# Attention over V in one full-precision matmul, or in three reduced-precision products with V and the probabilities split

## The chip, the cores and the metric

The kernel runs on one core of a Trainium2 chip. The metric is the device time of one execution in microseconds (us). The core has five engines that run their own instruction streams and meet only at semaphores: PE (matmuls, with its weight loads, PEld), DVE (vector), ACT (scalar), POOL (GpSimd) and SP, which here only issues DMAs.

## The reference

The program is an attention over chunks followed by two feed-forward networks. Cut to what matters here:

```python
for c in range(nc):                                   # chunks of 32 queries
    k_full = concat(mem_k, k[l_start:r_end])          # 8 memory rows + up to 56 rows
    v_full = concat(mem_v, v[l_start:r_end])
    scores = scale * q_c @ k_full.T
    a = exp(scores - max(scores)); a = a / (sum(a) + 1e-9)
    out[c] = a @ v_full                               # <- the product that is changed
x = out as (3072 tokens, 512)
g = s * relu(x @ w_in)**2 + b;   x2 = g @ w_out       # first network, d_ff 2048
g2 = h * sigmoid(1.702 h), h = x2 @ w_in2; out = g2 @ w_out2   # second network
```

There are 4 batches x 8 heads of 768 tokens with 64 channels each.

## The kernel before

Attention works on 32 query tiles of 96 tokens (`QT`). For each tile the 120 key rows of its window and the 8 memory rows make a context of 128. Two heads share one unit of work, since 2 x 64 channels fill 128 partitions: 4 units (`HP`) per tile, 128 units in all. Units 0 to 15 are done in a start-up of their own; the other 112 (from `FIRST` = 16) run hidden inside the first network, and only they are touched by the change.

The matmuls of the networks take three products in the type fp32r in place of one in fp32: each operand is split into a high part, which is the fp32 value converted to fp32r, and a low part, the value less the high part, and the products are high x high, high x low, low x high. ACT makes the high parts (`Copy` into an fp32r tile), DVE or POOL the low ones (a subtraction). In the steady attention, before the change, the scores are made in this way (`score`, L830, 3 matmuls of 256 columns), while the product with V is one fp32 matmul (`attend`, L853) of 192 columns (two heads x 96 tokens). In the trace an fp32 matmul is two records. The transposes (L817, L818, L841) are fp32 too.

The first network runs over token tiles `mm` 0 to 4, of 384, 384, 384, 480 and 480 tokens (`SIZES`). Each tile has 16 steps `f`. A step has 24 places: 12 matmuls of `first_product` (L885) and 12 of `second_product` of two steps earlier (L910 and L912). The table `AT` hangs the attention work onto these places. A unit n has a group of kind 1 and, some places later, one of kind 2; I call the two together a beat. PE in kind 1: transposes of the probabilities of unit n+1 (`transpose_probs`, L841), transposes of Q and K of unit n+4 (`transpose_qk`, L817 and L818). PE in kind 2: `attend(n)` and `score(n+3)`. There is about one beat per 19 places in tile 0, one per 16 in tiles 1 and 2, one per 12 (so two in a step) in tile 3, and one per 13.5 in tile 4 up to its ninth step.

ACT, in kind 1: `exp(n+2)` (L1071, two heads), `split_qk_hi(n+4)` (L1065, three pieces); in kind 2: `copy_x_hi(n)` (L1092 or L1097), and for units below 32 also `normalize` (L1078). Between them stand the step's own `nonlinear` (L1117, at place 12), `split_g_hi` (L1125) and in tile 0 `split_w_out_hi` (L1134). DVE in kind 1: `invert(n+2)` (L1412, L1416), `split_qk_lo(n+4)` (L1396, three pieces), `copy_pT(n+1)` (L1423, the transposed probabilities from PSUM to SBUF); in kind 2: `mask_and_max(n+3)` (L1405, two heads), `split_x_lo(n)` (L1428 or L1433); and the step's `gate` (L1458) and `split_g_lo` (L1464). POOL splits the weights in tile 0 (L646, L648, L653) and normalizes from unit 32 on (L695). Bank 6 of PSUM holds the transposed Q and K and the transposed probabilities, bank 7 the scores and the attention's output.

Every engine works its stream in order. `transpose_probs(n+1)` waits for the probabilities of its unit, for `pT_ready` of unit n (the copy out of bank 6) and for `qk_ready` of unit n+3 (the last L1396). SP issues the loads: Q and K of a tile (L471 to L474), V (`load_v`, L479 and L480) into one of two buffers `v_steady`, and the weights of tile 0 (L507, L516). `load_steady_v(j)` waits until the last unit of tile j-2 is attended, and what stands behind it in SP's queue waits with it.

## Time and profile before

| | us |
|---|---|
| median of 3 runs | 1174.82 (1174.70 to 1174.91) |
| the profiled execution | 1174.82 |
| its span, first to last instruction | 1173.0 |
| PE busy | 1162.9 (99%) |
| PE weight loads | 1016.2 (87%) |
| DVE busy | 905.1 (77%) |
| ACT busy | 670.8 (57%) |
| POOL busy | 348.6 (30%) |
| granted TensorE clock | 1.000 |

The profile is of one execution, whose own time is the median of the runs. Busy time of an engine is the union of its instructions; on PE an instruction's record lasts longer than the time until the next one may start, because the array is pipelined. So starts are compared below, not durations, where the pace of PE is meant. Steady attention lies between about 30 and 476 us; after it the two networks run alone.

### The profile page before, as it was taken

How to read it: one execution, taken by the hardware profiler on the slowest of the kernel's cores; microseconds unless marked ns; L12 is line 12 of the kernel's file. 1: busy time of each engine (PE TensorE's matmuls, PEld its weight loads, DVE VectorE, ACT ScalarE, POOL GpSimd, SP SyncE). 2: the span in 40 equal slices, each digit the busy share in tenths (PEclk: the TensorE clock that was granted, in tenths of full speed). 3: DMA queues.
4: the chain of work that ended last, by engine and by line, in shares of the span. 5: the costliest groups of instructions: out<-in, count | busy, mean ns of one | idle time of the engine just before them, and what ended most of it. 6: DMA issues, size and time to landing. Idle time of an engine off the chain costs nothing.

```text
span 1173.0 us, 19116 instructions
## 1 busy us (share of the span) xinstructions
PE 1162.9 (99%) x6058; PEld 1016.2 (87%) x6058; DVE 905.1 (77%) x2261; ACT 670.8 (57%) x1795; POOL 348.6 (30%) x356
## 2 busy tenths in 40 slices
PE   8999999999999999999999999999999999999998
PEld 5899999999988888888888888888888888888887
DVE  6788877878887887668898877879577878677663
ACT  6788766767766766345446554447344556444452
POOL 3754111111111111324642134640246421244300
PEclk9999999999999999999999999999999999999999
DMA  7753322322242231113424434124233234222231
GB/s 151 166 134 77 78 57 58 78 57 51 52 81 66 50 99 36 37 36 107 144 75 123 123 106 141 57 76 140 77 104 126 76 106 133 82 71 73 73 116 63
DMA packets 167689, 104.26 MB, mean 89 GB/s; under 512 B 99495, under 2 KB 144039, under 8 KB 167591
## 3 DMA queue, kind: packets, MB, share of 16 engines
q1 hardware_dynamic: 166368, 102.82, 32.5%
q8 instruction: 50, 0.82, 0.3%
q14 instruction: 48, 0.39, 0.1%
q10 hardware_dynamic: 1223, 0.23, 0.1%
HBM read 89.26 MB, written 13.76 MB: 88 GB/s over the span
## 4 chain that ended last, share of the span: by engine, by line
PE 95%; ACT 2%; DVE 1%; DMA 1%; issue 0%; POOL 0%; SPq 0%; POOLq 0%; DVEq 0%
PE psum L953 26%; PE psum L910 22%; PE psum L912 22%; PE psum L885 14%; PE psum L830 3%; PE psum L853 3%; PE psum L841 2%; PE psum L818 1%; DMA result<-in_moe_w_out_dram 1%; PE psum L817 1%; PE psum L752 1%; ACT arena_raw L1071 0%; PE psum L789 0%; PE psum L779 0%; ACT arena_raw L1078 0%
## 5 line engine op out<-in xcount | busy, mean ns | idle before, releaser
L953 PE MATMUL psum<-weights 128*128 128x512 f32 (+1 forms) x1344 | 337.6, 386 | 0.0
L953 PEld LDWEIGHTS psum<-weights 128*128 128x128 f32 x1344 | 252.3, 188 | 49.1
L912 PE MATMUL psum<-g_hi,weights 128*128 128x384 f32 (+1 forms) x768 | 223.3, 363 | 0.0
L885 PE MATMUL psum<-arena,weights 128*128 128x384 f32 (+1 forms) x960 | 215.7, 360 | 0.0
L1501 DVE TENSOR_TENSOR arena_raw<-psum,arena_raw 128x512 f32<-128x512 f32 (+1 forms) x160 | 109.0, 681 | 85.6 <-PE psum L953 83.7
L885 PEld LDWEIGHTS psum<-arena,weights 128*128 128x128 f32 x960 | 166.3, 188 | 8.8 <-DVE ffn L1458 0.2
L695 POOL TENSOR_TENSOR arena_raw<-arena_raw,small 96x256 f32<-96x256 f32 x96 | 58.6, 610 | 302.8 <-DVE small L1416 302.8
L912 PEld LDWEIGHTS psum<-g_hi,weights 128*128 128x128 f32 x768 | 139.3, 188 | 8.8
L912 PE MATMUL psum<-g_lo,weights 128*128 128x384 f32 (+1 forms) x384 | 138.2, 360 | 0.0
L910 PE MATMUL psum<-weights,g_hi 128*128 128x512 f32 x384 | 118.2, 389 | 0.0
L665 POOL TENSOR_TENSOR arena_raw<-arena_raw 128x256 f32<-128x256 f32 x32 | 27.2, 851 | 305.7 <-DMA arena_raw<-in_moe_w_in_dram 187.7
L1187 ACT ACTIVATE arena_raw<-arena_raw 128x512 f32<-128x512 f32 x48 | 30.4, 633 | 128.6 <-DVE arena_raw L1501 128.6
L1396 DVE TENSOR_TENSOR arena<-psum,arena 128x96 fp32r<-128x96 f32 x336 | 82.9, 274 | 24.8 <-ACT arena L1065 20.6
L1071 ACT ACTIVATE arena_raw<-arena_raw,small 96x128 f32<-96x128 f32 x224 | 87.4, 392 | 25.2 <-DVE small L1405 25.1
L658 POOL TENSOR_TENSOR weights<-arena_raw,weights 128x512 fp32r<-128x512 f32 x48 | 69.1, 1453 | 86.1 <-ACT weights L1146 86.1
L910 PEld LDWEIGHTS psum<-weights,g_hi 128*128 128x128 f32 x384 | 72.1, 188 | 15.0
L1471 DVE TENSOR_TENSOR weights<-arena_raw,weights 128x1024 fp32r<-128x1024 f32 x64 | 83.5, 1305 | 0.0
L1146 ACT ACTIVATE weights<-arena_raw 128x512 fp32r<-128x512 f32 x96 | 58.5, 625 | 39.4 <-PE psum L910 26.7
L1065 ACT ACTIVATE arena<-psum 128x96 fp32r<-128x96 f32 x336 | 75.0, 257 | 4.1 <-PE psum L818 1.6
L912 PEld LDWEIGHTS psum<-g_lo,weights 128*128 128x128 f32 x384 | 72.1, 188 | 5.5
L910 PE MATMUL psum<-weights,g_lo 128*128 128x512 f32 x192 | 74.7, 389 | 0.0
L910 PE MATMUL psum<-weights,arena 128*128 128x512 f32 x288 | 74.5, 389 | 0.0
(129 smaller groups left out, 2124.3 us busy)
## 6 DMA issues: line engine op xcount, KB each, us to landing
arena_raw<-in_moe_w_out_dram SPq DMA_DIRECT2D x128, 256.0 KB, 4.0
arena_raw<-in_moe_w_in_dram SPq DMA_DIRECT2D x64, 256.0 KB, 3.1
arena_raw<-in_k_dram SPq DMA_DIRECT2D x31, 240.0 KB
arena_raw<-in_v_dram SPq DMA_DIRECT2D x30, 240.0 KB
arena_raw<-x_scratch SPq DMA_DIRECT2D x3, 2048.0 KB, 10.5
arena_raw<-in_q_dram SPq DMA_DIRECT2D x31, 192.0 KB
out_dram<-result SPq DMA_DIRECT2D x5, 1024.0 KB, 5.1
result<-in_moe_w_in_dram SPq DMA_DIRECT2D x16, 256.0 KB, 4.2
```

The source lines that it names most:

```text
L658: nc.gpsimd.tensor_tensor(lo, w_out_raw(k), hi.bitcast(F32), ALU.subtract).then_inc(w_out2_now_ready, 1)
L695: nc.gpsimd.tensor_tensor(probs[:, n % 2, :, :], probs[:, n % 2, :, :], inv_total[:, n % 2, :].unsqueeze(2).to_broadcast([QT, 2, P]), ALU.mult
L885: last = nc.tensor.matmul(dst, w[:, kt * P:(kt + 1) * P], x, start=(kt + i == 0), stop=(kt == KT - 1 and i == 2))
L910: last = nc.tensor.matmul(acc[c][:, :], g[:, piece], w, start=start, stop=stop)
L912: last = nc.tensor.matmul(acc[c][:, 0:n], w[:, piece], g, start=start, stop=stop)
L953: last = nc.tensor.matmul(bank_of[bank][:, 0:width(i)], w[:, k * P:(k + 1) * P], x[:, k, :], start=(k + t == 0), stop=(k == 1 and t == 2))
L1065: last = nc.scalar.activation(qk_hi[parts, n % 2, cols], bank_qk[parts, source], ACT.Copy)
L1071: nc.scalar.activation(probs[:, n % 2, h, :], probs[:, n % 2, h, :], ACT.Exp, scale=-1.0, bias=exp_bias[:, n % 2, h:h + 1], accum_out=tota ...
L1146: nc.scalar.activation(hi, w_out_raw(k), ACT.Copy).then_inc(w_out2_hi_done, 1)
L1396: last = nc.vector.tensor_tensor(qk_lo[parts, n % 2, cols], bank_qk[parts, source], qk_hi[parts, n % 2, cols].bitcast(F32), ALU.subtract)
L1471: last = nc.vector.tensor_tensor(rows_parts(q, 1)[:, these], rows_raw[:, these], rows_parts(q, 0)[:, these].bitcast(F32), ALU.subtract)
L1501: return nc.vector.tensor_tensor(to[:, 0:w], bank_of[bank][:, 0:w], other[:, 0:w], ALU.add)
```

## The change

The product with V is done as the scores are: V and the transposed probabilities are split into high and low parts, and `attend` issues three fp32r matmuls of 192 columns in place of one fp32 matmul.

- V is loaded into one raw buffer, `v_raw`. POOL splits it: `split_v(j)` is a conversion of 128x512 and a subtraction of 128x512 per query tile, 28 tiles in all. It stands in POOL's stream once ahead of the tiles, and then once per tile at kind 1 of the unit with n % 4 == 1, behind `normalize(n+2)` where there is one.
- ACT gets one more instruction per unit, `split_pT_hi(n+1)`, 128x192 from PSUM, behind `split_qk_hi(n+4)` in kind 1.
- DVE's `copy_pT` becomes `split_pT_lo`, a subtraction of the same size. `split_qk_lo(n+4)` now waits for `pT_hi_done` of unit n+1 as well.
- `max_ready` is raised once per unit, not once per head, and `exp` waits for it ahead of both heads.
- SP: `load_steady_v(j)` waits for `v_ready` of tile j-1 (the split of the tile before, by POOL) in place of `attended` of tile j-2; the very first one waits for `s_attended` 6.

Cut to its core, the diff is:

```diff
-        pT = raw_area(ATTN + 4480, 384).rearrange("p (a c) -> p a c", a=2)
-        v_steady = raw_area(ATTN + 5248, 1024).rearrange("p (a c) -> p a c", a=2)
+        pT_hi = area(ATTN + 4480, 384).rearrange("p (a c) -> p a c", a=2)
+        pT_lo = area(ATTN + 4864, 384).rearrange("p (a c) -> p a c", a=2)
+        v_hi = area(ATTN + 5248, 1024).rearrange("p (a c) -> p a c", a=2)
+        v_lo = area(ATTN + 6272, 1024).rearrange("p (a c) -> p a c", a=2)
...
             def load_steady_v(j):
-                if HP * (j - 2) >= FIRST:
-                    sp.wait_ge(attended, nth(HP * (j - 1) - 1))
-                load_v(j, v_steady[:, j % 2, :], v_loaded[j % 2])
+                if HP * (j - 1) < FIRST:
+                    sp.wait_ge(s_attended, 2 * ((FIRST // HP - 1) // 2 * 2 + 1))
+                else:
+                    sp.wait_ge(v_ready, nth(HP * j - 1) // HP)
+                load_v(j, v_raw, v_loaded)
...
+            def split_v(j):
+                i = j - FIRST // HP
+                pool.wait_ge(v_loaded, 32 * (i + 1))
+                if i >= 2:
+                    pool.wait_ge(attended, nth(HP * (j - 1) - 1))
+                nc.gpsimd.tensor_copy(v_hi[:, j % 2, :], v_raw).then_inc(v_hi_done, 1)
+                pool.wait_ge(v_hi_done, i + 1)
+                nc.gpsimd.tensor_tensor(v_lo[:, j % 2, :], v_raw, v_hi[:, j % 2, :].bitcast(F32), ALU.subtract
+                                        ).then_inc(v_ready, 1)
...
+            split_v(FIRST // HP)
...
                         for kind, n in AT.get(pos, ()):
+                            j = n // HP + 1
                             if kind == 1 and there(n + 2) and pool_normalizes(n + 2):
                                 normalize(n + 2)
+                            if kind == 1 and n % HP == 1 and there(HP * j) and j > FIRST // HP:
+                                split_v(j)
...
                 if hp == 0:
-                    pe.wait_ge(v_loaded[j % 2], 32 * ((j - FIRST // HP) // 2 + 1))
+                    pe.wait_ge(v_ready, j - FIRST // HP + 1)
                 pe.wait_ge(pT_ready, nth(n))
-                nc.tensor.matmul(bank_o, v_steady[:, j % 2, hp * P:(hp + 1) * P], pT[:, n % 2, :], start=True, stop=True
-                                 ).then_inc(attended, 1)
+                for i, (a, c) in enumerate(((v_hi, pT_hi), (v_hi, pT_lo), (v_lo, pT_hi))):
+                    last = nc.tensor.matmul(bank_o, a[:, j % 2, hp * P:(hp + 1) * P], c[:, n % 2, :],
+                                            start=(i == 0), stop=(i == 2))
+                last.then_inc(attended, 1)
...
+            def split_pT_hi(n):
+                if there(n + LEAD - 1):
+                    act.wait_ge(qk_transposed, nth(n + LEAD - 1))
+                act.wait_ge(probs_transposed, nth(n))
+                nc.scalar.activation(pT_hi[:, n % 2, :], bank_pT, ACT.Copy).then_inc(pT_hi_done, 1)
             def exp(n):
+                act.wait_ge(max_ready, nth(n))
                 for h in range(2):
-                    act.wait_ge(max_ready, 2 * nth(n) - 1 + h)
...
             def split_qk_lo(n):
                 dve.wait_ge(qk_hi_done, nth(n))
+                if there(n - LEAD + 1):
+                    dve.wait_ge(pT_hi_done, nth(n - LEAD + 1))
...
-            def copy_pT(n):
-                if there(n + LEAD - 1):
-                    dve.wait_ge(qk_transposed, nth(n + LEAD - 1))
-                dve.wait_ge(probs_transposed, nth(n))
-                nc.vector.tensor_copy(pT[:, n % 2, :], bank_pT).then_inc(pT_ready, 1)
+            def split_pT_lo(n):
+                dve.wait_ge(pT_hi_done, nth(n))
+                nc.vector.tensor_tensor(pT_lo[:, n % 2, :], bank_pT, pT_hi[:, n % 2, :].bitcast(F32), ALU.subtract
+                                        ).then_inc(pT_ready, 1)
```

ACT's stream in a step of tile 3, from the step's `nonlinear` over its second beat. Before:

```order
L1117 ACTIVATE ffn<-psum 128x480 [waits hid_ready]
L1071 ACTIVATE arena_raw,small<-arena_raw,small 96x128 [waits max_ready] x2
L1065 ACTIVATE arena<-psum 128x96 [waits qk_transposed]
L1065 ACTIVATE arena<-psum 64x128 x2
L1092 ACTIVATE result<-psum 64x96 [waits result_stored,attended,scored]
```

and after, where L1149 is L1117 of before, L1101 is L1071, L1088 is L1065, L1122 is L1092, and L1096 is `split_pT_hi`:

```order
L1149 ACTIVATE ffn<-psum 128x480 [waits hid_ready]
L1101 ACTIVATE arena_raw,small<-arena_raw,small 96x128 [waits max_ready]
L1101 ACTIVATE arena_raw,small<-arena_raw,small 96x128
L1088 ACTIVATE arena<-psum 128x96 [waits qk_transposed]
L1088 ACTIVATE arena<-psum 64x128 x2
L1096 ACTIVATE arena<-psum 128x192 [waits probs_transposed,qk_transposed]
L1122 ACTIVATE result<-psum 64x96 [waits result_stored,attended,scored]
```

One instruction came in between L1065 and the copy of the attention's output.

DVE's stream in a beat of a tile of 384 tokens. Before:

```order
L1412 TENSOR_SCALAR small<-small 96x2 [waits exp_done]
L1416 RECIPROCAL small<-small 96x2 [waits probs_ready,total_ready]
L1396 TENSOR_TENSOR arena<-psum,arena 128x96 [waits qk_hi_done]
L1396 TENSOR_TENSOR arena<-psum,arena 64x128 x2
L1423 COPY arena_raw<-psum 128x192 [waits probs_transposed,qk_transposed]
L1464 SCALAR_TENSOR_TENSOR g_lo<-ffn,columns,g_hi 128x384 [waits g_hi_done]
```

and after:

```order
L1446 TENSOR_SCALAR small<-small 96x2 [waits exp_done]
L1450 RECIPROCAL small<-small 96x2 [waits probs_ready,total_ready]
L1430 TENSOR_TENSOR arena<-psum,arena 128x96 [waits pT_hi_done,qk_hi_done]
L1430 TENSOR_TENSOR arena<-psum,arena 64x128 x2
L1454 TENSOR_TENSOR arena<-psum,arena 128x192 [waits pT_hi_done]
L1496 SCALAR_TENSOR_TENSOR g_lo<-ffn,columns,g_hi 128x384 [waits g_hi_done]
```

The number and the places of the instructions are the same; the first subtraction, and with it all behind it, now stands behind ACT's new instruction.

POOL's stream where tile 0 begins. Before:

```order
L646 CAST weights<-result 128x512 [waits w_in_loaded0]
L648 TENSOR_TENSOR weights<-result,weights 128x512 [waits w_hi_first_in]
L646 CAST weights<-result 128x512 [waits w_in_loaded1]
L648 TENSOR_TENSOR weights<-result,weights 128x512 [waits w_hi_first_in]
L653 TENSOR_TENSOR weights<-result,weights 128x512 [waits w_hi_out]
```

and after:

```order
L653 CAST weights<-result 128x512 [waits w_in_loaded0]
L655 TENSOR_TENSOR weights<-result,weights 128x512 [waits w_hi_first_in]
L705 CAST arena<-arena_raw 128x512 [waits v_loaded]
L707 TENSOR_TENSOR arena<-arena_raw,arena 128x512 [waits v_hi_done]
L653 CAST weights<-result 128x512 [waits w_in_loaded1]
L655 TENSOR_TENSOR weights<-result,weights 128x512 [waits w_hi_first_in]
L660 TENSOR_TENSOR weights<-result,weights 128x512 [waits w_hi_out]
```

The two instructions of the first V stand between the second and the third piece of `w_in` that POOL converts.

## Rows read from the trace of the kernel before

**Rows 1.** The page: the chain that ended last, share of the span by engine.

```profile
PE 95%; ACT 2%; DVE 1%; DMA 1%; issue 0%; POOL 0%; SPq 0%; POOLq 0%; DVEq 0%
```

**Rows 2.** By stage (tile 0; tiles 1 and 2; tile 3); (x) counts.

```profile
core 0: us, PE busy (x) PEld busy (x) DVE busy (x) ACT busy (x) POOL busy (x), PEclk, DMA share, GB/s
30.00:113.00 83.00, 80.13 (x510) 76.04 (x511) 66.67 (x237) 67.72 (x234) 49.31 (x46) 1.00 0.57 133
113.00:305.00 192.00, 192.00 (x1246) 190.11 (x1246) 155.11 (x657) 131.68 (x509) 30.16 (x50) 1.00 0.29 60
305.00:427.00 122.00, 121.53 (x705) 108.03 (x704) 100.29 (x423) 82.00 (x321) 20.46 (x34) 1.00 0.34 72
```

**Rows 3.** Timeline, tile 2: start us, us, engine, line, tiles, count.

```profile
251.45 0.49 PE L853 MATMUL psum<-arena_raw 128*128 128x192 f32 x2
...
251.64 0.65 PE L830 MATMUL psum<-arena 128*96 128x256 f32 x3
251.84 0.36 DVE L1423 COPY arena_raw<-psum 128x192 f32<-128x192 f32 x1
...
252.13 0.69 PE L885 MATMUL psum<-arena,weights 128*128 128x384 f32 x3
```

**Rows 4.** Timeline, tile 0: scores without a product with V before them.

```profile
41.83 0.52 PE L830 MATMUL psum<-arena 128*96 128x256 f32 x3
...
42.19 0.34 PE L912 MATMUL psum<-g_lo,weights 128*128 128x384 f32 x1
```

**Rows 5.** Timeline, start-up: weight loads of fp32r matmuls of 128 columns.

```profile
15.76 0.58 PEld L779 LDWEIGHTS psum<-arena 64*96 64x96 f32 x12
```

**Rows 6.** Single lines, weight loads: duration ns min/median/max, first and last start, forms.

```profile
L779 PEld LDWEIGHTS psum<-arena x96: 156/162/162, 7.3 to 27.5; 64*96 64x96 f32 x96
...
L912 PEld LDWEIGHTS psum<-g_hi,weights x768: 187/188/193, 40.8 to 674.0; 128*128 128x128 f32 x192
```

**Rows 7.** Timeline, tile 3: the second beat of a step.

```profile
343.89 0.57 ACT L1117 ACTIVATE ffn<-psum 128x480 f32<-128x480 f32 x1 [1.06 <-PE psum L885]
...
345.12 0.68 ACT L1065 ACTIVATE arena<-psum 128x96 fp32r<-128x96 f32 x3
...
346.62 0.36 DVE L1423 COPY arena_raw<-psum 128x192 f32<-128x192 f32 x1
...
347.11 0.38 PE L912 MATMUL psum<-g_lo,weights 128*128 128x480 f32 x1
347.20 0.14 PEld L841 LDWEIGHTS psum<-ident,arena_raw 96*128 96x128 f32 x1
...
347.23 0.28 DVE L1405 CUSTOM_DVE_ANT_0 arena_raw<-psum,masks 96x128 f32<-96x128 f32 x1
```

**Rows 8.** Single lines of the start-up that have the size of the new ones.

```profile
L1059 ACT ACTIVATE arena<-psum x8: 306/310/332, 15.4 to 34.0; 128x192 fp32r<-128x192 f32 x8
...
L1390 DVE TENSOR_TENSOR arena<-psum,arena x8: 356/358/360, 15.8 to 34.4; 128x192 fp32r<-128x192 f32 x8
```

**Rows 9.** Timeline, tile 2: the transposes behind the copy of rows 3.

```profile
253.36 0.33 PEld L841 LDWEIGHTS psum<-ident,arena_raw 96*128 96x128 f32 x2
```

**Rows 10.** Timeline, tile 0: ACT, and PE behind it.

```profile
98.67 0.50 ACT L1097 ACTIVATE arena<-psum 64x96 fp32r<-64x96 f32 x2
...
99.95 0.20 PEld L841 LDWEIGHTS psum<-ident,arena_raw 96*128 96x128 f32 x2 [0.38 <-ACT arena_raw L1078]
```

**Rows 11.** What SP waited for up to 120 us: us, times, longest.

```profile
SPq L479 <- PE psum L853: 37.8, 4, 13.7
```

**Rows 12.** Timeline, end of tile 0: the first unit that POOL normalizes.

```profile
112.19 0.61 POOL L695 TENSOR_TENSOR arena_raw<-arena_raw,small 96x256 f32<-96x256 f32 x1 [0.29 <-DVE small L1416]
...
114.03 0.32 PEld L841 LDWEIGHTS psum<-ident,arena_raw 96*128 96x128 f32 x2
```

**Rows 13.** Timeline, tile 0: a small DVE instruction beside one of POOL.

```profile
41.20 1.28 POOL L653 TENSOR_TENSOR weights<-result,weights 128x512 fp32r<-128x512 f32 x1
41.23 1.28 DVE L1412 TENSOR_SCALAR small<-small 96x2 f32<-96x2 f32 x1 [0.42 <-ACT arena_raw L1071]
```

More of the change, by code:

```diff
@@ L324, in bass_chunked_attention_two_ffn @@
         s_v_loaded = [sem("s_v_loaded0"), sem("s_v_loaded1")]
-        v_loaded = [sem("v_loaded0"), sem("v_loaded1")]
+        v_loaded = sem("v_loaded")
+        v_hi_done = sem("v_hi_done")
+        v_ready = sem("v_ready")
         w_in_loaded = [sem("w_in_loaded0"), sem("w_in_loaded1")]
@@ L357, in bass_chunked_attention_two_ffn @@
         probs_transposed = sem("probs_transposed")
+        pT_hi_done = sem("pT_hi_done")
         pT_ready = sem("pT_ready")
@@ L825, in score @@
                 if there(n - 1):
-                    pe.wait_ge(max_ready, 2 * nth(n - 1))
+                    pe.wait_ge(max_ready, nth(n - 1))
                 if there(n - LEAD):
@@ L848, in attend @@
                 if there(n + LEAD - 2):
-                    pe.wait_ge(max_ready, 2 * nth(n + LEAD - 2))
+                    pe.wait_ge(max_ready, nth(n + LEAD - 2))
                 if hp == 0:
-                    pe.wait_ge(v_loaded[j % 2], 32 * ((j - FIRST // HP) // 2 + 1))
+                    pe.wait_ge(v_ready, j - FIRST // HP + 1)
                 pe.wait_ge(pT_ready, nth(n))
-                nc.tensor.matmul(bank_o, v_steady[:, j % 2, hp * P:(hp + 1) * P], pT[:, n % 2, :], start=True, stop=True
-                                 ).then_inc(attended, 1)
+                for i, (a, c) in enumerate(((v_hi, pT_hi), (v_hi, pT_lo), (v_lo, pT_hi))):
+                    last = nc.tensor.matmul(bank_o, a[:, j % 2, hp * P:(hp + 1) * P], c[:, n % 2, :],
+                                            start=(i == 0), stop=(i == 2))
+                last.then_inc(attended, 1)
             def group(kind, n):
@@ L1107, in group @@
                         split_qk_hi(n + LEAD)
+                    if there(n + 1):
+                        split_pT_hi(n + 1)
                 else:
@@ L1404, in mask_and_max @@
                 for h in range(2):
-                    nc.vector.tensor_tensor_reduce(
+                    last = nc.vector.tensor_tensor_reduce(
                         out=probs[:, n % 2, h, :], in0=bank_s[0:QT, h * P:(h + 1) * P], in1=masks[:, mask_of(n // HP), :],
-                        scale=-SCALE, scalar=-MASKED, op0=ALU.add, op1=ALU.min, accum_out=exp_bias[:, n % 2, h:h + 1]
-                        ).then_inc(max_ready, 1)
+                        scale=-SCALE, scalar=-MASKED, op0=ALU.add, op1=ALU.min, accum_out=exp_bias[:, n % 2, h:h + 1])
+                last.then_inc(max_ready, 1)
             def invert(n):
@@ L1445, in group @@
                     if there(n + 1):
-                        copy_pT(n + 1)
+                        split_pT_lo(n + 1)
                 else:
```

## The prediction

> **What bounds the kernel now.** I read the chain that ended last first. It is PE for 95% of the span [rows 1], so a microsecond that PE gains or loses is one of the result. Then the busy time by stage [rows 2]. While attention runs beside tiles 1 and 2, PE is busy for 192.00 of 192 us, in tile 3 for 121.53 of 122, and in tile 0 for 80.13 of 83. ACT is busy there for 131.68, 82.00 and 67.72 us, and DVE for 155.11, 100.29 and 66.67, which is about 80%. The granted clock is 1.00 in all of them, its higher level. So PE is the bound and the others feed it, with little room left. What the change is worth is therefore two things: what the three products take on PE, and whether ACT's new instruction makes a wait of PE's longer. After 480 us nothing of it is left in the program.
>
> **PE: the products.** One product with V and one group of scores take from 251.45 to 252.13, 0.68 us [rows 3]. Scores alone take from 41.83 to 42.19, 0.36 us, or 120 ns for each fp32r matmul of 256 columns [rows 4]. So the fp32 product costs 0.32 us. The new one is three fp32r matmuls of 192 columns with 128 columns of weights, a form that the trace does not have. By their columns they would start every 90 ns (192/256 of 120). But each has a weight load of its own. The start-up's matmuls stream 128 columns over a load of 96 columns, in pairs on the two halves of the rows: 12 loads in 0.58 us, the last lasting 0.162. That is 0.418 us over five pair intervals, 84 ns each [rows 5, 6], where their columns would give 60. There the load sets the pace. A load of 128 columns lasts 188 ns against 162 [rows 6], 26 ns more, so I expect 110 ns between starts. Behind the third comes a load of only 96 columns, so 90 ns. Together 110 + 110 + 90 = 310 ns against 320: 10 ns saved, x 112 units = 1.1 us. The bounds are 3 x 90 = 270 ns (5.6 us saved) and, since a matmul of 256 columns takes no more than 120, 3 x 120 = 360 (4.5 us lost). I take 310, nearest to the row of the small matmuls.
>
> A load of 128 columns of fp32r lasts 26 ns longer than one of 96 [rows 6], in line with its width and with no sign of a faster way at the full width. The Trainium skill, page "TensorE: Matmul & The Clock Gate", section "Weight-path perf modes — Fast Weight Load (FWL) and DoubleRow", has weights of exactly 128 columns load about twice as fast where the type is not FP32. By that rule the load would hide and the product would cost 270 ns, 5.6 us saved in all; the trace's row speaks against it for fp32r.
>
> **ACT and DVE.** `split_pT_hi` has the size of the start-up's L1059: 0.31 us. `split_pT_lo` has that of L1390, 0.358 us [rows 8], against 0.36 for the copy that it replaces [rows 3]. So DVE's own work stays, but all of its L1396 and what follows moves back by 0.31 us, since the first L1396 now waits for ACT's new instruction. What waits behind it on DVE is the last part of the beat: L1396, the low part, and then the maxima of the next unit. PE waits for these at L841.
>
> In tile 3 there is no room for it. ACT starts the second beat when PE's products release L1117 at 343.89. L1065 runs from 345.12 to 345.80 behind it, DVE's copy ends at 346.98, and the load of L841 starts at 347.20. The copy's end is thus passed on in 0.22 us. PE's last matmul ahead began at 347.11 and one of 480 columns takes about 0.22 more, so PE came to L841 at 347.33 [rows 7]: the room is 0.13 us at most, and I take 0.1. This repeats in each of the 16 steps of the tile. The wait starts from PE's own products of the same step, so nothing makes up for it in the next: 16 x (0.31 - 0.10) = 3.4 us. Bounds: 0, if ACT makes up for it, and 16 x 0.31 = 5.0.
>
> In tiles 1 and 2 the copy ends at 252.20 [rows 3] and L841's load starts at 253.36 [rows 9]: 1.16 us, less 0.22 for passing it on, leaves 0.94. The change wants 0.31, and 0.21 for `exp`, which now waits for the second head's maximum too (one head's pass is recorded at 0.28 [rows 7], and the two overlap a little). This is hidden. For the two beats behind the result copies, where DVE is late, and for tile 4, I add 0.4 us; bounds 0 and 2.
>
> In tile 0 ACT also normalizes and splits `w_out`, and PE waits for the normalizing: L1097 from 98.67, and its load for L841 waits 0.38 us for that, until 99.95 [rows 10]. ACT is busy for 67.72 of 83 us [rows 2] and gets 17 x 0.31 = 5.3 more. I take 8 of the 17 beats as having no idle time of ACT in them: 2.5 us, and 0.4 for two in which `exp` starts late. Bounds 0 and 5.3 + 0.8.
>
> **POOL and SP.** `split_v` has a subtraction of the size of L653, 1.28 us [rows 13], and a conversion that I take at half of it, as it reads one input: 1.9 us per query tile. From tile 1 on POOL is idle for 162 of 192 us [rows 2], and V is wanted three beats later: nothing. At one place it counts. The split of the ninth query tile stands between the last L653, which ends 0.29 us ahead of 112.19, and the first L695 [rows 12]. L695 then ends near 111.90 + 1.9 + 0.61 = 114.4, while PE loads for L841 at 114.03: 0.5 us late, once. On SP, `load_v` waited for PE for 37.8 us in all, up to 13.7 at a time, with the loads of weights behind it [rows 11]. The new wait, for a split that stands about 1.5 beats ahead in the program, is shorter where POOL is early. I take 0.4 us as gained in tile 0 (0 to 1.5), since the PE waits there are partly for late `w_out`.
>
> **The sum.** -1.1 (products) + 3.4 (tile 3) + 0.4 + 2.5 + 0.4 + 0.5 - 0.4 = +5.7 us. The profiled execution took 1174.82 us (span 1173.0), which is also the median, so 1180.5 us. This case's own range is 1177.5 to 1185.
>
> **Rivals.**
> 1. The three products run at their columns' pace, 270 ns, and the waits come as above. -5.6 in place of -1.1: 1176.0 us. For it: PE loads ahead of time everywhere else. Against it: the 84 ns of rows 5.
> 2. Faster: the products at 270 ns, and the waits do not appear, because ACT has 30 to 40% of idle time and starts its beat earlier than I think. Then 1174.8 - 5.6 + 0.7 (what is left in tile 0) = 1169.9 us. Decided where L841 waits in tile 3: below 0.05 us per step. Against it: L1065 there is back to back with the work ahead of it.
> 3. DVE is held by POOL. A DVE instruction of two elements lasts 1.28 us beside a POOL subtraction, almost start to end [rows 13]. `split_v` adds 28 such subtractions, most of them where POOL was idle. If 10 of them catch a small DVE instruction or L1464 and push it by 0.9 us of which 0.7 reaches PE, 7 us more: 1187.5 us. For it: rows 13. Against it: in tiles 1 and 2 there is 0.4 us of room left, and `split_v` follows L695, when DVE works from PSUM.
> 4. Tile 0 is starved of weights: the splits of V and SP's new first waits delay `w_in` by 2 us more than I think, and PE waits 3 us or more: 1184 us.
>
> The wait on L1412 of rows 13 is what the Trainium skill describes on its page "SBUF — State Buffer", section "SBUF: two separate sides", as the port pair that DVE and GpSimd take in turns, each for a whole instruction. The trace agrees (1.28 us beside 1.28), and the rule gives nothing for the sum beyond rival 3.
>
> **Chances.** My forecast 0.50, rival 1 0.17, rival 2 0.14, rival 3 0.12, rival 4 0.07. A measurement can tell 0.2% from no change, 2.35 us here. Slower than 1177.2: 0.45 of mine, all of rivals 3 and 4, and 0.03 of rival 1: 0.67. Within: 0.05 + 0.14 = 0.19. Faster: 0.14. For the range I reach to rival 3 above and to just short of rival 2 below: 1171 to 1189 us.
>
> **What would show it.** The new matmuls' weight loads should start 110 ns apart; 90 speaks for rivals 1 and 2, 120 or more against my step on PE. In tile 3 the L841 of the second beat should start 0.2 us later against the matmul ahead of it, and the stretch from the tile's first to last matmul should be 3.4 us longer. In tiles 1 and 2 PE should keep a busy share of 100% and their stretch shrink by 0.5 us (48 x 10 ns). In tile 0 the idle time of PE should grow by about 3 us. Stretched instructions L1412 and L1464 in tiles 1 to 3, now at their plain durations, would show rival 3. I am wrong if tile 3 does not get longer, or if the products' pace is off by more than 15 ns.

## The result, and the profile after

The changed kernel takes 1192.37 us (median of 4 runs, 1191.92 to 1192.62) against 1174.87 for the kernel before on the same chip: 1.47% slower, ratio 1.0147 with the interval 1.013 to 1.0165. Its profiled execution took 1191.04 us, span 1189.2. My 1180.5 had the direction and missed two thirds of the size; the time lies outside my range.

The page of the changed kernel: busy time, and the chain that ended last, which answers to [rows 1].

```profile
PE 1170.7 (98%) x6170; PEld 1010.4 (85%) x6170; DVE 895.9 (75%) x2261; ACT 698.6 (59%) x1907; POOL 401.2 (34%) x412
...
PE 85%; ACT 6%; DVE 4%; issue 3%; POOL 1%; DVEq 0%; ACTq 0%; POOLq 0%
```

PE's share of the chain falls from 95% to 85%. ACT and DVE have taken seven of these ten points and `issue` three, though ACT's busy share only went from 57 to 59% and DVE's fell from 77 to 75%. It is their order that the kernel waits for, not their load. By stage, with windows moved to where the stages now lie; this answers to [rows 2].

```profile
core 0: us, PE busy (x) PEld busy (x) DVE busy (x) ACT busy (x) POOL busy (x), PEclk, DMA share, GB/s
30.00:114.00 84.00, 80.20 (x524) 75.74 (x525) 65.27 (x236) 70.36 (x248) 57.19 (x55) 1.00 0.57 132
114.00:312.00 198.00, 195.76 (x1293) 186.28 (x1292) 150.84 (x654) 142.19 (x550) 53.43 (x75) 1.00 0.27 60
312.00:440.00 128.00, 123.18 (x729) 104.96 (x728) 94.61 (x422) 90.63 (x354) 34.72 (x49) 1.00 0.28 66
```

The clock is at its higher level as before. PE, which had no gap in tiles 1 and 2, has 2.2 us of them now, and 4.8 in tile 3 (0.5 before). A better measure is how late `transpose_probs` (L841, now L862) of a given unit starts. Unit 33, at the end of tile 0, starts at 120.09 us against 118.77; unit 81, at the end of tile 2, at 311.39 against 303.62; unit 113, at the end of tile 3, at 435.49 against 420.27. So tile 0 costs 1.3 us, tiles 1 and 2 cost 6.5 in their 48 beats, tile 3 costs 7.4 in its 32, and the rest 0.9. I had 3.0, 0.4 (with tile 4) and 3.4. This one execution is 1.3 us faster than the median; no trace shows where the others lose that.

The groups of ACT and DVE in tiles 1 and 2, first before (118 to 305 us), then after (ACT from 118 to 312, DVE from 118 to 305): busy time, mean of one | idle time ahead of them and what ended it.

```profile
L1405 DVE CUSTOM_DVE_ANT_0 arena_raw<-psum,masks 96x128 f32<-96x128 f32 x98 | 24.4, 284 | 11.9 <-ACT arena L1097 9.0 <-ACT result L1092 1.6
L1071 ACT ACTIVATE arena_raw<-arena_raw,small 96x128 f32<-96x128 f32 x98 | 38.2, 391 | 8.1 <-DVE small L1405 8.1
L1097 ACT ACTIVATE arena<-psum 64x96 fp32r<-64x96 f32 x72 | 17.6, 244 | 30.6 <-PE psum L830 30.1
```

```profile
L1439 DVE CUSTOM_DVE_ANT_0 arena_raw<-psum,masks 96x128 f32<-96x128 f32 x94 | 23.0, 280 | 0.1
L1101 ACT ACTIVATE arena_raw<-arena_raw,small 96x128 f32<-96x128 f32 x96 | 37.8, 395 | 44.4 <-DVE small L1439 44.4
L1127 ACT ACTIVATE arena<-psum 64x96 fp32r<-64x96 f32 x74 | 18.0, 243 | 2.5 <-PE psum L851 1.8
L1430 DVE TENSOR_TENSOR arena<-psum,arena 128x96 fp32r<-128x96 f32 x141 | 35.0, 275 | 32.3 <-ACT arena L1096 31.5
```

These lines tell most of the case. Before, `copy_x_hi` on ACT waited 30.6 us for PE's scores, and the maxima 11.9 us, most of them for that copy, so in the end for PE as well. Now DVE hardly waits ahead of the maxima (0.1 us), and ACT and DVE wait for each other: `exp` 44.4 us for the maxima, `split_qk_lo` 32.3 us for `split_pT_hi`. A beat of tile 2:

```profile
243.72 0.28 DVE L1439 CUSTOM_DVE_ANT_0 arena_raw<-psum,masks 96x128 f32<-96x128 f32 x1
...
244.26 0.40 ACT L1101 ACTIVATE arena_raw<-arena_raw,small 96x128 f32<-96x128 f32 x1 [0.81 <-DVE small L1439]
...
245.05 0.67 ACT L1088 ACTIVATE arena<-psum 128x96 fp32r<-128x96 f32 x3
245.17 0.47 PE L875 MATMUL psum<-arena 128*128 128x192 f32 x3
...
245.48 0.52 PE L851 MATMUL psum<-arena 128*96 128x256 f32 x3
...
245.74 0.33 ACT L1096 ACTIVATE arena<-psum 128x192 fp32r<-128x192 f32 x1
245.84 1.56 PE L908 MATMUL psum<-arena,weights 128*128 128x384 f32 x8
...
246.17 0.76 DVE L1430 TENSOR_TENSOR arena<-psum,arena 128x96 fp32r<-128x96 f32 x3 [0.59 <-ACT arena L1096]
...
246.96 0.36 DVE L1454 TENSOR_TENSOR arena<-psum,arena 128x192 fp32r<-128x192 f32 x1
247.23 0.28 DVE L1439 CUSTOM_DVE_ANT_0 arena_raw<-psum,masks 96x128 f32<-96x128 f32 x1
247.39 0.20 PEld L862 LDWEIGHTS psum<-ident,arena_raw 96*128 96x128 f32 x2 [0.31 <-issue]
```

It is a ring: maxima (243.72), `exp` (244.26), high Q and K (245.05), high probabilities (245.74), low Q and K (246.17), low probabilities (246.96), and at once the maxima of the next unit (247.23). PE's transposes hang on it. In two of three beats a `split_g_lo` or a `gate` stands between the low probabilities and the next maxima besides; this is the third. In numbers, the change lengthens the ring by 0.22 us for `exp` (it starts 0.54 us behind the maxima; 0.32 in `b1_act` of the next section, where it waits for one head) and by 0.42 at `split_pT_hi` (from the end of the last L1088, 245.72, to L1430 at 246.17; before, from L1065's end, 239.49, to 239.51). The lines of `b1_act`, and those of the kernel before:

```profile
241.36 0.28 DVE L1417 CUSTOM_DVE_ANT_0 arena_raw<-psum,masks 96x128 f32<-96x128 f32 x1
...
241.68 0.40 ACT L1079 ACTIVATE arena_raw<-arena_raw,small 96x128 f32<-96x128 f32 x1 [0.68 <-DVE small L1417]
```

```profile
238.81 0.68 ACT L1065 ACTIVATE arena<-psum 128x96 fp32r<-128x96 f32 x3
...
239.51 0.76 DVE L1396 TENSOR_TENSOR arena<-psum,arena 128x96 fp32r<-128x96 f32 x3
```

### The profile page after: what moved, and what is told of

It is laid out like the page before. It is cut to its first block, busy times and chain, and to the rows that moved or that the text cites. A ratio compares the mean times of both kernels' runs of the same rounds, so it can differ in the third digit from the quotient of the medians.

```text
span 1189.2 us, 19643 instructions
## 1 busy us (share of the span) xinstructions
PE 1170.7 (98%) x6170; PEld 1010.4 (85%) x6170; DVE 895.9 (75%) x2261; ACT 698.6 (59%) x1907; POOL 401.2 (34%) x412
## 4 chain that ended last, share of the span: by engine, by line
PE 85%; ACT 6%; DVE 4%; issue 3%; POOL 1%; DVEq 0%; ACTq 0%; POOLq 0%
PE psum L976 25%; PE psum L933 22%; PE psum L935 18%; PE psum L908 11%; PE psum L851 2%; PE psum L875 2%; DVE arena L1430 2%; ACT arena_raw L1101 2%; PE psum L862 2%; ACT arena L1088 2%; ACT arena L1096 1%; PE psum L839 1%; DVE arena L1454 1%; PE psum L838 1%; PE psum L773 1%
## 5 line engine op out<-in xcount | busy, mean ns | idle before, releaser
L908 PE MATMUL psum<-arena,weights 128*128 128x384 f32 (+1 forms) x960 | 215.9, 360 | 0.2 <-DVE ffn L1490 0.2
L908 PEld LDWEIGHTS psum<-arena,weights 128*128 128x128 f32 x960 | 166.4, 188 | 9.1 <-DVE ffn L1490 0.4
L712 POOL TENSOR_TENSOR arena_raw<-arena_raw,small 96x256 f32<-96x256 f32 x96 | 58.6, 610 | 271.7 <-DVE small L1450 261.3
L1430 DVE TENSOR_TENSOR arena<-psum,arena 128x96 fp32r<-128x96 f32 x336 | 83.2, 275 | 68.3 <-ACT arena L1096 65.9
L1101 ACT ACTIVATE arena_raw<-arena_raw,small 96x128 f32<-96x128 f32 x224 | 88.0, 394 | 78.0 <-DVE small L1439 77.6
L1088 ACT ACTIVATE arena<-psum 128x96 fp32r<-128x96 f32 x336 | 74.7, 256 | 2.3
```

The source lines that it names most:

```text
L712: nc.gpsimd.tensor_tensor(probs[:, n % 2, :, :], probs[:, n % 2, :, :], inv_total[:, n % 2, :].unsqueeze(2).to_broadcast([QT, 2, P]), ALU.mult
L908: last = nc.tensor.matmul(dst, w[:, kt * P:(kt + 1) * P], x, start=(kt + i == 0), stop=(kt == KT - 1 and i == 2))
L1088: last = nc.scalar.activation(qk_hi[parts, n % 2, cols], bank_qk[parts, source], ACT.Copy)
L1101: nc.scalar.activation(probs[:, n % 2, h, :], probs[:, n % 2, h, :], ACT.Exp, scale=-1.0, bias=exp_bias[:, n % 2, h:h + 1], accum_out=tota ...
L1430: last = nc.vector.tensor_tensor(qk_lo[parts, n % 2, cols], bank_qk[parts, source], qk_hi[parts, n % 2, cols].bitcast(F32), ALU.subtract)
```

## The experiments

Four theories. **Ring**: what is added to the ring is paid once its room, the time that a turn has to spare against PE's beat, is used up. **Exp wait**: the wait for both heads is the price. **POOL**: `split_v` slows DVE down. **Products**: they are slower than thought. The table at the end of this section has where each kernel lost its time. Each time is compared with the kernel before on the same chip. The diffs are cut to the lines that matter, some of their conditions left out, and comments in them are mine.

**Parts put on the kernel before.** `b1_act`: ACT's operation and DVE's wait alone.

```diff
+            def copy_pT_spare(n):   # behind split_qk_hi(n + LEAD) in kind 1
+                act.wait_ge(probs_transposed, nth(n))
+                nc.scalar.activation(pT_spare[:, n % 2, :], bank_pT, ACT.Copy).then_inc(pT_hi_done, 1)
             def split_qk_lo(n):
+                    dve.wait_ge(pT_hi_done, nth(n - LEAD + 1))
             def copy_pT(n):
+                dve.wait_ge(pT_hi_done, nth(n))
```

> The kernel before, with one thing added: ACT's Copy of the transposed probabilities (128x192 from PSUM, into a place that nobody reads) behind split_qk_hi in kind 1, and DVE's split_qk_lo and copy_pT wait for it. V, the product and the two max_ready waits are as before. Ring theory (the extra ACT operation and its hand-over lengthen the closed loop maxima, exp, high Q and K, low Q and K, copy, next maxima by about 0.4 us a beat, and what a beat is late the next beat inherits): most of the 17.5 us returns here, +10 to +15 us on the kernel before, about 1185 to 1190. If exp's wait for both heads is the main price: +3 us or less. If POOL's work beside DVE is the price: 0. If the room of 0.94 us per beat hid it, as my prediction had it: +3 to +6, nearly all of it in tiles 0 and 3.

1183.59 us, +9.0 (ratio 1.0078, 1.0063 to 1.0093): just short of the ring's +10, above the others'. Nearly all of it is in tiles 0 (2.1) and 3 (5.9), with only 0.7 in tiles 1 and 2. That is where my prediction's room of 0.94 us would have put it too, so this run alone does not decide.

`b2_once`: the wait of `exp` alone.

```diff
-                    act.wait_ge(max_ready, 2 * nth(n) - 1 + h)
+            act.wait_ge(max_ready, nth(n))   # once, and max_ready raised once per unit
```

> The kernel before, with one thing changed: max_ready is raised once per unit behind the second head, and exp waits for it ahead of both heads. Ring theory: exp starts up to one maximum (0.31 us) later only where it had waited for the first head; in the kernel before the loop in tiles 1 and 2 still had room of about 0.5 us a beat, so +1 to +3 us, mostly in tile 3. If the exp wait is the main price of the change: +8 or more. If the waits are nothing and POOL or PE's pace is the price: 0.

1176.32, +1.7 (1.0005 to 1.0024). This is not the main price by itself. Its trace has all of it in tile 0, not in tile 3 as I expected.

`b3_pool`: POOL's conversion and subtraction per tile alone (`split_v` of the change, into `v_spare`).

```diff
+                nc.gpsimd.tensor_copy(v_spare[:, 0, :], v_steady[:, j % 2, :]).then_inc(v_hi_done, 1)
+                nc.gpsimd.tensor_tensor(v_spare[:, 1, :], v_steady[:, j % 2, :], v_spare[:, 0, :].bitcast(F32), ALU.subtract).then_inc(v_ready, 1)
```

> The kernel before, with POOL's two operations of 128x512 per query tile added (conversion and subtraction into places that nobody reads), at the places where the change puts split_v, and SP waits for them ahead of the load that would overwrite their input. Nothing else waits for them. Ring theory: 0 to +2 us, since only POOL's own queue is later (its normalize, once per tile, by up to 1 us). Rival, POOL's reads and writes slow DVE down: +7 us or more, and DVE's busy time up.

1177.09, +2.5 (1.001 to 1.003), a little above the ring's window and far from the rival's. Nearly all of it is in tile 0; in tiles 1 to 3 nothing. Yet its trace shows the contention there:

```profile
250.94 1.29 POOL L704 TENSOR_TENSOR arena<-arena_raw,arena 128x512 fp32r<-128x512 f32 x1
251.14 1.50 DVE L1482 SCALAR_TENSOR_TENSOR g_lo<-ffn,columns,g_hi 128x384 fp32r<-128x384 f32 x1
```

`split_g_lo` lasts 1.50 us in place of 0.62 and ends 0.41 us behind POOL's subtraction. The room swallows it: none of the four such places in tiles 1 and 2 makes a transpose late.

`b4_act_once`: both of the first two.

> The kernel before with both additions to the loop together: ACT's extra Copy with DVE waiting for it, and exp waiting for both heads. PE's product with V is still one fp32 matmul and POOL has no more work. Ring theory: the loop is as long as in the changed kernel and only the products' small gain is missing, so 1190 to 1195, the changed kernel's 1192.4 within 3 us. If the rest of the change (V split on POOL, three products, the later loads by SP) has a share of its own, it is short of that by this share: 1183 or less.

1199.09, +24.5 (1.0194 to 1.0224). The parts alone are +9.0 and +1.7; together they are more than twice their sum, and more than the whole change. That they don't add up speaks for a ring with room: in tiles 1 and 2 they cost 0.7 and 0.0 alone and 9.3 together. But I had expected no more than 1195, so something in the changed kernel must give 7 us back.

**Parts taken from the changed kernel.** `a1_heads`: `exp` waits head by head again.

> The changed kernel with max_ready raised per head again and exp waiting head by head. Ring theory: the loop is shorter by 0.1 to 0.2 us a beat where exp waits, so 1186 to 1189. If the exp wait is the main price of the change: 1180 or less. If POOL contention or the products are the price: 1192, no change.

1182.66, 9.7 us back, where I had thought of 3 to 6. Tiles 1 and 2 lose only 0.3 now, tile 3 still 5.8. The same wait that costs 1.7 us on the kernel before is worth 9.7 here.

`a3_pT_first`: ACT's order.

```diff
+                    if there(n + 1):
+                        split_pT_hi(n + 1)
                     if there(n + 2) and there(n):
                         exp(n + 2)
                     if there(n + LEAD) and there(n):
                         split_qk_hi(n + LEAD)
-                    if there(n + 1):
-                        split_pT_hi(n + 1)
```

> The changed kernel with ACT's split_pT_hi(n+1) moved ahead of exp(n+2) and split_qk_hi(n+4) in kind 1. ACT idles about 0.8 us there, waiting for the maxima, and the transposed probabilities are usually ready by then. Ring theory: the 0.33 us and its hand-over leave the loop, so most of the loss is back: 1174 to 1181. If the maxima wait no longer for it but exp's wait for both heads or POOL is the price: above 1187. If the probabilities are transposed too late for it, exp is held up by it and the kernel is slower than 1192.

1178.83 (1.0025 to 1.0055): 13.5 us back by moving one ACT instruction into ACT's idle time. The ring theory's window.

`a5_first_heads`: both.

> The changed kernel with both: split_pT_hi ahead of exp in ACT's stream, and exp waiting head by head. Ring theory: the loop is then as long as in the kernel before but for a DVE subtraction in place of a copy, and PE has the products' gain of 1.1 us less POOL's and the start's cost: 1173 to 1178. If something outside the loop costs, it stays above 1180.

1178.38, just outside. Tiles 1 and 2 are 0.4 us faster than before, tile 3 loses 2.8. There the transposes are as late as the maxima:

```profile
352.77 0.20 PEld L862 LDWEIGHTS psum<-ident,arena_raw 96*128 96x128 f32 x2 [0.25 <-issue]
...
353.09 0.28 DVE L1439 CUSTOM_DVE_ANT_0 arena_raw<-psum,masks 96x128 f32<-96x128 f32 x1
...
353.43 0.33 ACT L1096 ACTIVATE arena<-psum 128x192 fp32r<-128x192 f32 x1
...
353.64 0.40 ACT L1101 ACTIVATE arena_raw<-arena_raw,small 96x128 f32<-96x128 f32 x1
```

`exp` is held until 353.64 by `split_pT_hi`, 0.55 us behind the maxima and not 0.32.

`a8_first_both`: DVE's low part moved up as well.

```diff
+                if there(n - LEAD):   # split_qk_hi: bank 6 is read by one engine at a time
+                    act.wait_ge(pT_ready, nth(n - LEAD + 1))
+                    if there(n + 1):   # DVE, kind 1: ahead of invert and split_qk_lo
+                        split_pT_lo(n + 1)
```

> As the last one, and DVE's split_pT_lo(n+1) stands ahead of invert(n+2) and split_qk_lo(n+4) as well, so that both halves of the split fall under exp; ACT's split_qk_hi then waits for it, since both read bank 6. Ring theory: the split of the probabilities leaves the loop altogether, which is then shorter than in the kernel before by the copy's 0.33 us a beat: 1171 to 1175, below the kernel before's 1174.9. If bank 6's order becomes the bound (split_qk_hi late behind the low part), 1178 or more.

1180.04, a miss on the ring theory's side, and in the range of its rival, the order of bank 6: in tile 3 `split_qk_hi` now idles 7.5 us in all for `split_pT_lo`. No further run tested this.

**The 7 us that were unexplained.** In `b4_act_once` the operation ahead of the maxima is a copy, in the changed kernel a subtraction of the same duration. `c1_two_operands` is `b4_act_once` with one line changed (below), and `c3_one_operand` the changed kernel with a copy in place of the subtraction, so that it leaves the low part of the probabilities out.

```diff
-                nc.vector.tensor_copy(pT[:, n % 2, :], bank_pT).then_inc(pT_ready, 1)
+                nc.vector.tensor_tensor(pT[:, n % 2, :], bank_pT, pT_spare[:, n % 2, :].bitcast(F32), ALU.max).then_inc(pT_ready, 1)
```

> The kernel before with ACT's extra Copy, DVE's wait for it and exp's wait for both heads (the one that took 1199.1), and DVE's copy_pT now made by a tensor_tensor of two operands (the larger of the value and ACT's copy of it) in place of tensor_copy. In the traces DVE's next instruction starts 0.03 us after a tensor_copy's end but 0.09 us before a tensor_tensor's end, so the loop should be 0.12 us a beat shorter: where it is saturated (48 beats of tiles 1 and 2, 30 of tile 3) that is about 9 us, so 1188 to 1192. If the form of the operation is nothing and the 6.7 us between that kernel and the changed one lie in the three products or the V split, it stays at 1197 or more.

> The changed kernel with DVE's split_pT_lo made by a tensor_copy in place of the subtraction (the low part of the probabilities is left out). By the same 0.12 us a beat in 78 saturated beats: 1199 to 1203, slower by 7 to 10 us with one operand less. If the form is nothing: 1192.

1187.99 and 1202.22: 11.1 us less and 9.8 more, as expected. DVE in `b4_act_once` and in `c1_two_operands`:

```profile
250.51 0.36 DVE L1436 COPY arena_raw<-psum 128x192 f32<-128x192 f32 x1
250.89 0.29 DVE L1417 CUSTOM_DVE_ANT_0 arena_raw<-psum,masks 96x128 f32<-96x128 f32 x1
```

```profile
246.03 0.36 DVE L1436 TENSOR_TENSOR arena_raw<-psum,arena 128x192 f32<-128x192 f32 x1
246.30 0.28 DVE L1417 CUSTOM_DVE_ANT_0 arena_raw<-psum,masks 96x128 f32<-96x128 f32 x1
```

From start to start these are 0.38 against 0.27 us. `q1_v_copy` makes POOL's second operation a copy in the changed kernel, and so leaves the low part of V out:

```diff
-                nc.gpsimd.tensor_tensor(v_lo[:, j % 2, :], v_raw, v_hi[:, j % 2, :].bitcast(F32), ALU.subtract
+                nc.gpsimd.tensor_copy(v_lo[:, j % 2, :], v_raw).then_inc(v_ready, 1)
```

> The changed kernel with the second of POOL's operations per tile a tensor_copy in place of the subtraction (the low part of V is left out). In the changed kernel's trace split_g_lo of DVE, both of whose inputs are in SBUF, takes 1.18 to 1.33 us in place of 0.62 in the four places of tiles 1 and 2 where POOL's subtraction runs beside it, and PE is 0.8 us later behind each. If that is a cause: 3 us or so less, 1188 to 1190. If it is absorbed as it is where POOL's work was added to the kernel before: 1191 to 1193. If POOL's contention is the main price: 1185 or less.

1188.52, 3.9 us less. First the changed kernel, then this one:

```profile
254.52 1.29 POOL L707 TENSOR_TENSOR arena<-arena_raw,arena 128x512 fp32r<-128x512 f32 x1
...
254.90 1.33 DVE L1496 SCALAR_TENSOR_TENSOR g_lo<-ffn,columns,g_hi 128x384 fp32r<-128x384 f32 x1
256.15 0.28 DVE L1439 CUSTOM_DVE_ANT_0 arena_raw<-psum,masks 96x128 f32<-96x128 f32 x1
```

```profile
254.99 0.63 DVE L1495 SCALAR_TENSOR_TENSOR g_lo<-ffn,columns,g_hi 128x384 fp32r<-128x384 f32 x1
255.54 0.28 DVE L1438 CUSTOM_DVE_ANT_0 arena_raw<-psum,masks 96x128 f32<-96x128 f32 x1
```

So POOL's contention is a real cause here, where the ring has no room, and costs nothing in tiles 1 to 3 of `b3_pool`. In tiles 1 and 2 of the changed kernel four of the twelve subtractions of V hold up a `split_g_lo`. Behind each of these four the transposes get 0.76 to 0.88 us later, against 0.18 to 0.20 at the same places without the subtraction: 2.5 us of the 3.9. A fifth, at 474.36 us in tile 4, costs 0.7.

`p1_products`: the products alone on the kernel before, all three with the high parts (the low parts are left out), and one conversion per tile on POOL for V.

```diff
-                nc.tensor.matmul(bank_o, v_steady[:, j % 2, hp * P:(hp + 1) * P], pT[:, n % 2, :], start=True, stop=True
+                for i in range(3):
+                    last = nc.tensor.matmul(bank_o, v_hi[:, j % 2, hp * P:(hp + 1) * P], pT[:, n % 2, :], start=(i == 0), stop=(i == 2))
```

> The kernel before with the product with V made by three fp32r matmuls of 192 columns (three times high V by high probabilities, low parts left out); DVE's copy_pT writes fp32r, POOL makes V's high part by one conversion per tile, PE waits for that. ACT, exp's waits and DVE's order are those before. Both theories of the loop: the products' gain of 10 ns a unit, 1.1 us in all, and up to 1 us of POOL's work in tile 0 against it, so 1173.5 to 1175.5. If the three products carry a share of the loss: above 1177.

1173.48, -1.0 (ratio 0.9993, 0.9984 to 1.0003, so not clear of zero). The products are no part of the loss.

**Operands or partitions.** Still open was why a copy costs 0.12 us more. The four kernels here change only the order of the three pieces in DVE's `split_qk_lo`. The third piece starts at partition 64.

```diff
-                for (parts, cols), source in QK_PIECES:
+                for (parts, cols), source in QK_PIECES[2:] + QK_PIECES[:2]:
```

> The kernel before with ACT's extra Copy, DVE's wait for it and exp's wait for both heads, DVE's copy still with one operand (the 1199.1 us kernel), but DVE's split_qk_lo does its three pieces in the order third, first, second, so that the last one before the copy starts at partition 0 and not at 64. If the 0.12 us behind the copy come from its one operand, only the copy's own start is earlier: 1190 to 1194. If they come from the partition where the last SBUF operand began (the copy reads none, so the maxima are compared with the piece at partition 64), both go, 0.23 us a beat: no loss left in tiles 1 and 2 and 4 us in tile 3, 1181 to 1185.

> The changed kernel with only that order of split_qk_lo's pieces. split_pT_lo then starts 0.1 us earlier against the piece ahead of it. Loop theory: 0.1 us a beat off a loop that is 0.13 us too long in tiles 1 and 2 and 0.24 in tile 3, so 7 to 8 us less, 1183 to 1186. If the order of the pieces is nothing: 1192.

> The changed kernel with split_pT_hi ahead of exp, exp waiting head by head (the 1178.4 us kernel), and that order of the pieces. It lost 2.8 us in tile 3, 0.09 us a beat, and gained 0.4 in tiles 1 and 2. Loop theory: the 0.1 us a beat takes the loss in tile 3 away, 1175 to 1176.5, as fast as the kernel before within what can be measured. If tile 3 is held by ACT or by the order of bank 6 instead: 1177.5 or more.

> The kernel before with only that order of the pieces. Its loop has room in every tile, so a shorter one gives nothing: within 0.5 us of the kernel before. If its loop were the bound in tile 3: 1 to 3 us less.

`d4_act_once_order` took 1178.66 with the one-operand copy: 20.4 us less than `b4_act_once`, more even than I expected. DVE there:

```profile
240.56 0.76 DVE L1408 TENSOR_TENSOR arena<-psum,arena 64x128 fp32r<-64x128 f32 x3 [0.59 <-ACT arena L1074]
241.24 0.34 DVE L1436 COPY arena_raw<-psum 128x192 f32<-128x192 f32 x1
241.50 0.27 DVE L1417 CUSTOM_DVE_ANT_0 arena_raw<-psum,masks 96x128 f32<-96x128 f32 x1
```

Copy and maxima both start before their predecessor's record ends: 0.26 us from start to start. It was not the number of operands but the partition at which the last one from SBUF began; the second operand of `c1_two_operands` begins at partition 0, and that is how it helped. `d2_after_order`: 1182.29, 10.1 us less than the changed kernel and a little more than expected. `d1_first_order`: 1174.97, ratio 1.0004 (0.9995 to 1.0013): the whole loss gone, with the change's arithmetic complete. POOL's split, its meetings with `split_g_lo` and SP's new waits are all still in this kernel, so they cost nothing that can be measured once the ring has room. `d3_before_order`: 1173.23, ratio 0.999 (0.9981 to 0.9999), the fastest of these kernels (its product with V is the one of the kernel before). Against my expectation of 0.5 us at most it gained 1.4; 0.7 of that had come by the end of tile 0 and 0.4 in tile 3, too little to be sure of a cause.

Time lost against the kernel before (starts of the transposes of units 33, 81 and 113 and the end, in one profiled execution of each):

| us | tile 0 | tiles 1, 2 | tile 3 | rest |
|---|---|---|---|---|
| the changed kernel | 1.3 | 6.5 | 7.4 | 0.9 |
| b1_act | 2.1 | 0.7 | 5.9 | -0.1 |
| b2_once | 1.6 | 0.0 | 0.1 | 0.0 |
| b3_pool | 2.8 | 0.0 | -0.1 | 0.8 |
| b4_act_once | 2.7 | 9.3 | 11.5 | 0.7 |
| a1_heads | 0.9 | 0.3 | 5.8 | 0.6 |
| a3_pT_first | 1.4 | -0.3 | 2.8 | 0.1 |
| a5_first_heads | 1.0 | -0.4 | 2.8 | 0.1 |
| a8_first_both | 0.5 | 0.8 | 3.6 | 0.2 |
| c1_two_operands | 1.8 | 3.8 | 7.6 | 0.0 |
| c3_one_operand | 3.9 | 11.3 | 11.5 | 1.5 |
| q1_v_copy | 2.6 | 4.1 | 7.5 | 0.2 |
| p1_products | -1.2 | -0.4 | -0.1 | -0.2 |
| d4_act_once_order | -0.7 | 0.4 | 4.0 | 0.0 |
| d2_after_order | 0.5 | 1.9 | 4.2 | 0.8 |
| d1_first_order | -0.1 | -0.5 | 0.6 | 0.1 |
| d3_before_order | -0.7 | 0.0 | -0.4 | 0.0 |

One number for the room makes the column of tiles 1 and 2. Their 48 beats lose 0.194 us each in `b4_act_once`, where 0.42 + 0.22 = 0.64 is added: room 0.45. In `c1_two_operands` 0.64 - 0.11 = 0.53 is added and 0.079 lost: 0.45. In `b1_act` 0.42 is added and next to nothing lost. And `d4_act_once_order` adds 0.64 - 0.22 = 0.42 and loses 0.01. These are means: `b4_act_once` mostly loses about 0.3 us in two of three beats and less than 0.1 in the third.

## Why the prediction was wrong, step by step

- **Products, -1.1 us: right.** In the beat above L875 starts at 245.17 and L851 at 245.48, 0.31 us as worked out. Product and scores together take 0.67 us, up to L908 at 245.84, against 0.68 before [rows 3]. `p1_products` gained 1.0, within the noise.
- **Tiles 1 and 2, "this is hidden", +0.4: the step that failed.** The 0.52 us that I took as wanted is close to what the runs show (0.53), but that is luck: I had 0.31 for ACT and 0.21 for `exp`; it is 0.42 and 0.22, less 0.11 that the subtraction gives back. The room was not 0.94 us but 0.45. I read it where PE waits, from the end of the copy to the load of L841 [rows 3, 9]. But DVE starts the next maxima as soon as the copy is done, and from them the next copy follows through `exp` and the splits, so the room is that of the whole ring. The row that shows it was there: in tiles 1 and 2 of the kernel before DVE idled 11.9 us ahead of the maxima, 0.24 a beat, well below the 0.52 wanted. The other half of the room lies mostly ahead of `exp`. By the mean starts of all beats of tiles 1 and 2, the maxima came 1.03 us behind the copy before and 0.75 in `b4_act_once`, which is 0.27 of room; `exp` came 0.46 behind the maxima where 0.32 would have done, since ACT was often not free, which is 0.13 more; and 0.03 lay ahead of `split_qk_hi`: 0.44 in all. What is missing in one beat is passed to the next, and so 0.08 us became 3.8 in the 48 beats of `c1_two_operands`. The changed kernel loses 6.5 there, 2.5 of them by POOL's contention.
- **Tile 3, +3.4: mechanism right, size half.** From one beat [rows 7] I took 0.31 us added, a room of 0.1 and one late beat per step, 0.21 a step. "Nothing makes up for it in the next" holds, and so does the one late beat: but for the first step the changed kernel loses 0.33 to 0.47 us in one of a step's two beats and at most 0.13 in the other. The term that was mis-sized is what is added. `exp` waits for the second head here as well, which I had left out of this tile, and `split_pT_hi` costs 0.42 us and not 0.31: with the 0.11 back, 0.53 is added. My own sum would then give 16 x (0.53 - 0.10) = 6.9; lost are 7.4 us, 0.46 a step. A room of 0.1 is itself only rough: `b1_act` and `d4_act_once_order` both add 0.42 and lose 5.9 and 4.0, and I cannot say why they differ.
- **Rival 3, POOL's contention, 0.12: a true part.** I priced it at 7 us with 10 meetings; it is 3.9, of which the traces show 3.2: 2.5 from four meetings in tiles 1 and 2, and 0.7 from the one in tile 4. My argument against it, 0.4 us of room left, fell with the room. The Trainium skill, page "SBUF — State Buffer", section "Who interferes with whom", says that a DVE instruction with two SBUF inputs contends with one of POOL that reads SBUF, and that one with at most one does not, outside the modes that use two ports. The traces agree: L1496 has two and lasts 1.33 us. L1490, with one of its inputs in PSUM, keeps its 0.61 us at the four places of tiles 1 and 2 where POOL's subtraction runs beside all of it.
- **Tile 0, +3.0: too much**, 1.3 in the profiled execution (2.6 in that of `q1_v_copy`, which has the same ring). Rival 4, a tile 0 that loses 3 us or more beyond this, did not show. The one place that I named came as told, `split_v` between the last weight split and L712, with PE 0.40 us late:

```profile
113.58 1.30 POOL L707 TENSOR_TENSOR arena<-arena_raw,arena 128x512 fp32r<-128x512 f32 x1
114.84 0.61 POOL L712 TENSOR_TENSOR arena_raw<-arena_raw,small 96x256 f32<-96x256 f32 x1
115.51 0.20 PEld L862 LDWEIGHTS psum<-ident,arena_raw 96*128 96x128 f32 x2 [0.40 <-POOL arena_raw L712]
```

  The rest of tile 0 I did not settle: POOL's work alone costs 2.8 us there, ACT's alone 2.1, and the whole change 1.3.
- **SP, -0.4**: not tested by itself. Up to 120 us SP waits 32.1 us ahead of V's loads in place of the 37.8 [rows 11], but 15.3 in place of 7.1 ahead of those of `w_out`. **Rivals 1 and 2** (products at 270 ns) are refuted by the 0.31 us.

The sum, as the runs give it: ring without contention `c1_two_operands` +13.5, contention +3.9, products -1.0: +16.4, against +17.5 measured. The last 1.1 stays open; single runs of the kernel before spread over 2.5 us (1173.3 to 1175.8), and its medians on the chips used over 0.4 (1174.48 to 1174.87).

DVE's wait for `pT_hi_done` ahead of `split_qk_lo` was not taken away alone: ACT and DVE would then read bank 6 at the same time, which the program keeps apart. What it costs by itself stays open.

## What to carry to other kernels

Two engines that work in order and hand to each other form a ring, and its room is the time that its members still spend on the outside (here DVE ahead of the maxima, in the end for PE's scores, and `exp` behind ACT's other work), not the slack at the point where the bound engine picks up. Add up what a change puts into the ring per turn: below the room it costs nothing, above it the excess is paid turn after turn, and costs that were free apart are paid together. A single instruction moved into an engine's idle time can be worth more than the arithmetic that it serves: one ACT move gave 13.5 us and the order of three DVE pieces 10.1.

## What the runs showed of the hardware

- DVE starts an instruction that waits for nothing about 0.07 to 0.09 us before the record of its predecessor ends, or 0.01 to 0.03 us behind it. Which one depends on the partition at which operands begin: behind the piece at partition 64 the next instruction is held, and a copy from PSUM, which reads nothing from SBUF, hands that hold on to the instruction behind it. The Trainium skill, page "VectorE: DVE Perf Modes", section "Two Vector instructions with no wait between them", states this comparison: an instruction is held where an input begins in another group of 32 partitions than the last read from the same memory did, and likewise for outputs. The runs agree, and price it: 0.11 us each, twice a beat, 20.4 us between `b4_act_once` and `d4_act_once_order`.
- Three short fp32r matmuls, each with 128 columns of weights of its own, do not run at the pace of their 192 columns, which I estimate at 90 ns from 120 ns for 256 columns [rows 4]. The three L875 and the first L851 start 0.09, 0.11 and 0.11 us apart (medians of 109 units), 0.31 in all. I put this down to the weight loads, which start 0.11 us apart; no run varied them.
- DVE's `split_g_lo`, begun while a POOL subtraction with both inputs in SBUF runs, ends 0.42 us behind POOL's (254.52 + 1.29 = 255.81 against 256.23). At all eight such places in tiles 1 and 2 of the changed kernel and of `b3_pool` the lag is 0.41 to 0.42 us, though the records last from 1.18 to 1.50, so it is held rather than slowed. Where it began first, at four places in tiles 1 and 2 of `a5_first_heads`, it kept its 0.61 us and POOL's subtraction took 1.71 in place of 1.29.
